# Gated attention and two mixers on one core: clamp and loads one pair further ahead, the first mixer's early weights in one piece

## The chip, the cores and the metric

One of the eight cores of one Trainium2 chip. A core has TensorE (PE in the profile; PEld is its weight load), VectorE (DVE), ScalarE (ACT), GpSimd (POOL) and SyncE (SP), which here issues all DMA transfers; they run on the core's 16 DMA engines. The metric is the time of one execution on the device in microseconds (us), median of several runs.

## The reference

A linear attention with a decay per channel, for 4 batches of 8 heads, 768 tokens, 48 channels a head, feeds two mixers:

```
f = 1 / (1 + exp(-f_logit))
for t in range(S):
    state = f[:, :, t, :, None] * state + einsum('bhd,bhe->bhde', k[:, :, t], v[:, :, t])
    y[:, :, t] = einsum('bhd,bhde->bhe', q[:, :, t], state)
x = y as [batch, token, 384]
theta = x @ w_theta
u = x + w_tok_r @ (x * cos(theta)) + w_tok_i @ (x * sin(theta))
x = u + relu(u @ w_ch)
h = relu(x @ w_in);  a, v = halves of h;  v normalised over channels
out = (a * (w_spatial @ v + b_spatial)) @ w_out
```

## The kernel before

The program has three parts, one after the other, with a barrier between them: `attention` (about the first 121 us), `token_mix` and `gated_net`. Only `attention` is changed. (A fourth, `attention_any_decay`, runs only if a flag says that the decays sum up to too much; here it is skipped.)

**Attention works on pairs of heads.** 32 heads make 16 pairs. A pair's rows (two heads of 48 channels, at partitions 0 to 47 and 64 to 111) stand over its 768 tokens, in 6 chunks of 128. A pair goes through these steps, each a function that issues instructions on one engine:

- SP: `load_f` (L231) loads the gate logits, `load_rest` k, q and v; `store` writes the pair's y from `y_sb` to the tensor `xT` in HBM.
- DVE: `keep_in_range` (L490), the clamp of `f_raw` from below. ACT: `neg_logs` (L314, L316), Exp and Ln into `csum`. DVE: `sums` (L498, L501), a copy of chunk starts and the running sum in `csum`. POOL: `sum_tops`.
- ACT: `decays` (L323, `w_dn`), `growths` (L338, `w_up`), `chunk_ends` (L330, `ends`). DVE: `scale_queries` (L516, `qs`), `scale_keys` (L527, `ks`).
- PE: `turn` (L382) transposes the keys, ACT's `keys_out` (L349) copies them out; `scores` (L400) makes the scores inside the chunks; DVE's `scores_out` (L535, `att`) masks half of them, ACT's `scores_copy` (L355) and POOL's `mask_scores` (L295) the other half; `states` (L418) makes the chunks' states, which DVE's `state_sums` (L545) scans; `attended` (L439) and `carried` (L449) add up y in PSUM; ACT's `y_out` (L362) copies it to `y_sb`.

**The order is a software pipeline written by hand.** `pipeline(eng, stages)` runs turns n = 0, 1, 2, ...; in turn n it issues for each (function, lag) of the engine's list the step of pair n - lag, in the order of the list. Turns 0 to 3 are unrolled, turns 4 to 15 are a loop over four turns each, and the rest is unrolled again. Engines issue in order and meet through semaphores: a step waits for its inputs and until its output buffer is free. `p.back(2)` in a wait is the pair that used the same of two buffers. `f_raw`, `k_raw`, `q_raw`, `csum`, `w_dn`, `w_up`, `ks`, `att` and `y_sb` have two buffers, `qs` and `v_raw` four. So `load_f` waits for the Exp two pairs back, `load_rest` for `ks` and `qs` two pairs back and y four pairs back, `y_out` for the store two pairs back.

**The first mixer's weights.** `w_raw` is a staging area for the mixers' weights, of which the first 4224 columns (theta and two sixths of the token mixing) are loaded during attention: `load_weights` (L248) issues one slice of 352 columns (176 KB) in each turn of the loop, twelve in all. With the last pair `theta_hi` on ACT waits for all of them and splits the theta weights into a high part, `theta_lo` on DVE makes the low part. The other weights are loaded by `token_mix`, 768 KB at a time.

Of the kernel before, what the change touches and what calls it, by code (L numbers as in the profile page):

```python
# [25 lines left out]
UNROLL = 4  # L26
# [13 lines left out]
WB_COLS = W_CH + DT * DMODEL  # L40

MIX_PART = 2 * SEQ
WB_EARLY = W_MIX + 2 * MIX_PART
WB_PART = WB_EARLY // (PAIRS - UNROLL)


W_IN_COLS = DT * DFF
# [63 lines left out]
def attention(nc, sems, waits_passed, flag, flag_ready, w_hi, w_lo, w_raw, wb_in, wb_hi, wb_lo, wB, qT, kT, fT, vC, xT):  # L111
# [5 lines left out]
    with ExitStack() as ctx:  # L117
# [75 lines left out]
        def last_pair(p):  # L193
            return p.reg is None and p.const == PAIRS - 1

        def pipeline(eng, stages, most=3):

            def steps(reg, consts, bounded):
                for n in consts:
                    for fn, lag in stages:  # L200
                        p = n - lag
                        if not bounded or 0 <= p < PAIRS:
                            fn(Step(reg, UNROLL, p), p % UNROLL)
            steps(None, range(UNROLL), True)
            with eng.Fori(0, PAIRS // UNROLL - 1) as it:
                steps(it, range(UNROLL, 2 * UNROLL), False)
            steps(None, range(PAIRS, PAIRS + most), True)

        def across(t, hd, c):
# [9 lines left out]
        @block.sync  # L219
        def _(sp):  # L220
            for c in x_out:
                c.open(sp)

            def rows(raw, src, name, sem, p, b):
                if p.reg is None and p.const < 2:
                    sp.wait_ge(cleared[name], b + 1)
                for hd in range(2):
                    sp.dma_start(raw[b % 2][HEAD_AT[hd]:HEAD_AT[hd] + HDIM, :],
                                 src[p.times(1), hd * HDIM:(hd + 1) * HDIM, :]).then_inc(sem[b % 2].h, 16)

            def load_f(p, b):  # L231
                sp.wait_ge(lg_done.h, lg_done.at(p.back(2), 1))
                rows(f_raw, fT, "f", f_in, p, b)

            def load_rest(p, b):
                sp.wait_ge(k_done.h, k_done.at(p.back(2), 1))
                rows(k_raw, kT, "k", k_in, p, b)
                sp.wait_ge(q_done.h, q_done.at(p.back(2), 1))
                rows(q_raw, qT, "q", q_in, p, b)
                sp.wait_ge(y_ps.h, y_ps.at(p.back(4), 2))  # L240
                sp.dma_start(v[b][:, :].rearrange("p (h x) -> p h x", h=2),
                             vC[p.times(1), :, :, :].rearrange("h p x -> p h x")).then_inc(v_in[b].h, 16)

            def load_weights(p, b):

                if p.reg is not None:
                    cols = bass.ds(p.times(WB_PART, -UNROLL * WB_PART), WB_PART)
                    sp.dma_start(w_raw[:, cols], wB[:, cols]).then_inc(wb_in, 16)  # L248

            def store(p, b):  # L250
                i = b % 2
                sp.wait_ge(y_sbd.h, y_sbd.at(p, 2))
                for hd in range(2):
                    sp.dma_start(xT[p.times(1), hd * HDIM:(hd + 1) * HDIM, :],
                                 y_sb[i][HEAD_AT[hd]:HEAD_AT[hd] + HDIM, :]).then_inc(x_out[i].h, 16)

            pipeline(sp, [(load_f, 0), (load_rest, 1), (load_weights, 0), (store, 4)], 4)
            for b in range(2):
                sp.wait_ge(x_out[b].h, 32 * (PAIRS // 2 + 1))

        @block.gpsimd
        def _(pool):
# [32 lines left out]
                    pool.affine_select(out=group, in_=group, compare_op=ALU.is_ge, fill=0.0, base=0,  # L295
                                       pattern=[[0, 3], [1, CHUNK]], channel_multiplier=-1).then_inc(a_sb.h, 1)

            pipeline(pool, [(sum_tops, 1), (mask_scores, 2)])

        @block.scalar  # L300
        def _(act):
# [37 lines left out]

            def theta_hi(p, b):  # L340
                if last_pair(p):
                    act.wait_ge(wb_in, 16 * (PAIRS - UNROLL))
                    split_hi(act, w_hi[:, W_THETA:W_MIX], w_raw[:, W_THETA:W_MIX]).then_inc(wb_hi, 1)

            def keys_out(p, b):
# [11 lines left out]
            def y_out(half):  # L357
                def f(p, b):
                    i = b % 2
                    act.wait_ge(x_out[i].h, half_count(x_out[i], p, 2) - 32)  # L360
                    act.wait_ge(y_ps.h, y_ps.at(p, half + 1))
                    act.activation(y_sb[i][:, half * 384:half * 384 + 384], y_ps_[half][0:ROWS, 0:384], ACT.Copy)\  # L362
                       .then_inc(y_sbd.h, 1)
                return f

            pipeline(act, [(neg_logs, 0), (keys_out, 2), (decays, 1), (growths, 1), (scores_copy, 2), (chunk_ends, 1), (theta_hi, 2), (y_out(0), 3), (y_out(1), 3)])

        @block.tensor
        def _(pe):
# [16 lines left out]
            def scores(half):  # L386
                def f(p, b):
                    i = b % 2
                    pe.wait_ge(q_done.h, q_done.at(p, 1))
                    pe.wait_ge(k_done.h, k_done.at(p, 1))  # L390
                    for hd in range(2):

                        if half == 0:
                            pe.wait_ge(a_masked.h, a_masked.at(p.back(1), hd + 1))
                        else:
                            pe.wait_ge(a_out.h, a_out.at(p.back(1), hd + 1))
                    for c in range(3 * half, 3 * half + 3):
                        for hd in range(2):
                            rows = slice(HEAD_AT[hd], HEAD_AT[hd] + HDIM)
                            last = pe.matmul(att_ps[2 * half + hd][:, (c % 3) * CHUNK:(c % 3 + 1) * CHUNK],  # L400
                                             ks[i][rows, c * CHUNK:(c + 1) * CHUNK],
                                             qs[b][rows, c * CHUNK:(c + 1) * CHUNK], start=True, stop=True)
                            if c % 3 == 2:
                                last.then_inc(a_ps.h, 1)
                return f
# [48 lines left out]
            def turn_tops(p, b):  # L454
                if last_pair(p):
# [3 lines left out]
                    pe.matmul(kt_ps_[0:1, 0:ROWS], top[:, :], ident[0:ROWS, 0:ROWS], start=True, stop=True)\  # L459
                      .then_inc(tops_turned, 1)  # L460

            pipeline(pe, [(turn, 2), (scores(0), 2), (scores(1), 2), (attended(0), 3), (attended(1), 3), (states, 2),
                          (carried(0), 3), (carried(1), 3), (turn_tops, 3)])
            last = Step(None, 1, PAIRS - 1)

            pe.wait_ge(a_masked.h, a_masked.at(last, 1))
# [4 lines left out]
        def _(dve):  # L471
# [57 lines left out]
            def scores_out(g):  # L529
                def f(p, b):  # L530
                    dve.wait_ge(y_ps.h, y_ps.at(p.back(2), 2))
                    dve.wait_ge(a_ps.h, a_ps.at(p, g + 1))
                    if first(p) and g == 0:
                        dve.wait_ge(const_ready, 5)
                    dve.tensor_tensor(att[b % 2][:, g * 384:(g + 1) * 384],  # L535
                                      view(att_ps[g], 0, [[CHUNK, 3], [1, CHUNK]]),
                                      view(causal, 0, [[0, 3], [1, CHUNK]]), ALU.mult).then_inc(a_masked.h, 1)
                return f
# [11 lines left out]
                    dve.wait_ge(wb_hi, 1)  # L550
                    split_lo(dve, w_lo[:, W_THETA:W_MIX], w_raw[:, W_THETA:W_MIX], w_hi[:, W_THETA:W_MIX]).then_inc(wb_lo, 1)

            pipeline(dve, [(keep_in_range, 0), (sums, 1), (scores_out(0), 2), (scores_out(1), 2), (scale_queries, 1), (scale_keys, 1), (state_sums, 2), (row_tops, 1), (theta_lo, 2)])
            dve.wait_ge(wb_lo, 1)

            dve.wait_ge(tops_turned, 1)
# [1412 lines left out]
```

## Time and profile before

| | us |
|---|---|
| median of 3 runs | 646.15 |
| lowest, highest | 645.97, 650.05 |
| the profiled execution's own time | 648.72 |
| its span, first to last instruction | 647.0 |
| PE busy over the span | 600.0 (93%) |
| DVE busy | 367.8 (57%) |
| ACT busy | 290.4 (45%) |
| mean granted clock of TensorE | 0.973 |

The profile is of one execution. Engine busy times are sums over the whole span; attention is a stage with other proportions than the mixers, and is read by itself. A row of the timeline is a run of instructions of one kind: start, duration, engine, line, output<-inputs, count, and in brackets how long the engine was idle before it and what ended that. "Us to landing" of a DMA is from its issue to the semaphore that says that it is done. The granted clock is a share of TensorE's full 2.4 GHz.

### The profile page before, as it was taken

What the parts mean: (1) busy time and instruction counts of PE and PEld (TensorE: products, weight loads), DVE (VectorE), ACT (ScalarE), POOL (GpSimd) and SP (SyncE); (2) the same over time, 40 slices, a digit from 0 to 9 for tenths busy, and PEclk for the clock granted to TensorE, in tenths of its full rate; (3) what the DMA queues carried; (4) which work ended last, traced back from release to release, by engine and by line L of the source; (5) the groups of instructions that cost most, each with busy time, mean ns of one, the idle gap of its engine ahead of it and who ended that gap; (6) DMA issues with size and microseconds to landing.
All of it is one profiled execution on the core that took longest, in us unless ns stands there. A gap on an engine that the chain in (4) does not pass through costs nothing. (4 is left out here: it accounts for less than half of the span.)

```text
span 647.0 us, 12122 instructions
## 1 busy us (share of the span) xinstructions
PE 600.0 (93%) x4262; PEld 574.4 (89%) x4262; DVE 367.8 (57%) x618; ACT 290.4 (45%) x513; POOL 31.5 (5%) x68
## 2 busy tenths in 40 slices
PE   1988989579979999999999989999999999999998
PEld 1877877469979999999999987999999899989998
DVE  6888999247677644845573363865505642463141
ACT  5877988245556323533442123632531343134112
POOL 2222223000000000000000000000000000000000
PEclk9996999969979999999999989999999999999999
DMA  8897997282041022102201413350022002000102
GB/s 187 184 255 214 252 257 198 58 291 77 25 146 50 25 62 98 37 36 64 83 12 37 146 63 135 108 162 0 2 74 74 0 0 73 0 0 14 62 0 74
DMA packets 33707, 58.77 MB, mean 91 GB/s; under 512 B 3968, under 2 KB 25984, under 8 KB 33664
## 3 DMA queue, kind: packets, MB, share of 16 engines
q1 hardware_dynamic: 33664, 58.21, 30.9%
q8 instruction: 25, 0.41, 0.3%
q14 instruction: 18, 0.15, 0.1%
HBM read 44.04 MB, written 14.16 MB: 90 GB/s over the span
## 5 line engine op out<-in xcount | busy, mean ns | idle before, releaser
L999 PE MATMUL mix_ps<-w_hi,z_hi 128*128 128x384 f32 x288 | 99.8, 346 | 2.4 <-DVE z_lo L78 2.4
L999 PE MATMUL mix_ps<-w_lo,z_hi 128*128 128x384 f32 x288 | 97.8, 340 | 0.0
L999 PE MATMUL mix_ps<-w_hi,z_lo 128*128 128x384 f32 x288 | 97.6, 339 | 0.0
L999 PE MATMUL gate_ps<-w_hi,w_lo 128*128 128x384 f32 x192 | 64.2, 334 | 0.0
L999 PE MATMUL gate_ps<-w_hi 128*128 128x384 f32 x192 | 64.1, 334 | 0.0
L999 PE MATMUL gate_ps<-w_lo,w_hi 128*128 128x384 f32 x192 | 64.1, 334 | 0.0
L999 PEld LDWEIGHTS mix_ps<-w_hi,z_hi 128*128 128x128 f32 x288 | 54.6, 190 | 3.6 <-issue 3.6
L999 PEld LDWEIGHTS mix_ps<-w_lo,z_hi 128*128 128x128 f32 x288 | 54.5, 189 | 0.0
L999 PEld LDWEIGHTS mix_ps<-w_hi,z_lo 128*128 128x128 f32 x288 | 54.4, 189 | 0.0
L73 ACT ACTIVATE g_hi<-gate 128x384 fp32r<-128x384 f32 x32 | 16.9, 527 | 76.0 <-DVE gate L1875 76.0
L1871 DVE TENSOR_TENSOR gate<-gate_ps,b_all 128x384 f32<-128x384 f32 x32 | 17.8, 557 | 56.8 <-PE gate_ps L999 56.4
L78 DVE TENSOR_TENSOR xt_lo<-xt,xt_hi 128x1152 fp32r<-128x1152 f32 x16 | 21.4, 1355 | 46.8 <-ACT xt_hi L73 46.8
L1445 DVE TENSOR_TENSOR z<-z,xn 128x384 f32<-128x384 f32 x48 | 24.7, 555 | 26.3 <-ACT z L1248 26.3
L1242 ACT ACTIVATE turns<-ang 128x384 f32<-128x384 f32 x24 | 12.7, 527 | 54.0 <-DVE ang L1433 54.0
L999 PEld LDWEIGHTS gate_ps<-w_lo,w_hi 128*128 128x128 f32 x192 | 36.0, 188 | 0.0
L999 PEld LDWEIGHTS gate_ps<-w_hi 128*128 128x128 f32 x192 | 36.0, 188 | 0.0
L999 PEld LDWEIGHTS gate_ps<-w_hi,w_lo 128*128 128x128 f32 x192 | 36.0, 188 | 0.0
L1231 ACT ACTIVATE turns<-theta_bank 128x384 f32<-128x384 f32 x24 | 11.7, 488 | 51.5 <-PE theta_bank L999 51.4
L999 PE MATMUL ringc<-xt_hi,in_hi 128*128 128x384 f32 x96 | 32.2, 336 | 0.5 <-ACT ut L1700 0.5
L999 PE MATMUL ringc<-w_hi,g_lo 128*128 128x384 f32 x96 | 32.2, 336 | 0.0
L999 PE MATMUL ringc<-w_hi,g_hi 128*128 128x384 f32 x96 | 32.2, 336 | 0.0
L999 PE MATMUL ringc<-w_lo,g_hi 128*128 128x384 f32 x96 | 32.2, 336 | 0.0
(129 smaller groups left out, 1390.1 us busy)
## 6 DMA issues: line engine op xcount, KB each, us to landing
f_raw<-in_fT_dram SPq DMA_DIRECT2D x32, 144.0 KB, 3.3
k_raw<-in_kT_dram SPq DMA_DIRECT2D x32, 144.0 KB, 3.7
q_raw<-in_qT_dram SPq DMA_DIRECT2D x32, 144.0 KB, 4.1
v_raw<-in_vC_dram SPq DMA_DIRECT2D x16, 288.0 KB, 4.5
xT<-y_sb SPq DMA_DIRECT2D x32, 144.0 KB, 2.9
xt<-xT SPq DMA_DIRECT2D x8, 576.0 KB, 4.1
u<-xT SPq DMA_DIRECT2D x8, 576.0 KB, 5.3
x2T<-x SPq DMA_DIRECT2D x24, 192.0 KB, 1.9
```

The costliest lines, as they stand in the source:

```text
L73: return act.activation(hi, x, ACT.Copy)
L78: return dve.tensor_tensor(lo, x, hi.bitcast(F32), ALU.subtract)
L999: done = pe.matmul(out, a, b, start=(first and n == 0), stop=(last and n == len(terms) - 1))
L1231: act.activation(turns[s % 2][:, :], theta_bank[:, 0:DMODEL], ACT.Copy, bias=MAGIC, scale=TURN_INV).then_inc(turns_done.h, 1)
L1242: act.activation(turns[i][:, :], ang[i][:, :], ACT.Abs).then_inc(mag_done.h, 1)
L1445: dve.tensor_tensor(z[i][:, cols], z[i][:, cols], part(xn, s * DMODEL, DMODEL), ALU.mult)\
L1871: dve.tensor_tensor(cols, gate_ps[g % 4][:, 0:HALF], part(b_all, th * HALF, HALF), ALU.add)\
```

## The change

Everything in `attention` but the loads of a pair and its clamp is issued one turn later. On DVE the clamp also leaves its place at the head of the turn and stands behind the masks of the scores. SP's loads keep their lags, its store goes from lag 4 to 5, and SP's unrolled part is eight turns long. The slices of weights leave the loop; three transfers of 1152, 1536 and 1536 columns are issued behind the loads of the last pair, ahead of a store.

```
-WB_EARLY = W_MIX + 2 * MIX_PART
-WB_PART = WB_EARLY // (PAIRS - UNROLL)
+WB_EARLY = [(W_THETA, W_MIX), (W_MIX, MIX_PART), (W_MIX + MIX_PART, MIX_PART)]
...
-        def pipeline(eng, stages, most=3):
+        def pipeline(eng, stages, most=4, lead=UNROLL):
...
-            steps(None, range(UNROLL), True)
-            with eng.Fori(0, PAIRS // UNROLL - 1) as it:
-                steps(it, range(UNROLL, 2 * UNROLL), False)
+            steps(None, range(lead), True)
+            with eng.Fori(0, (PAIRS - lead) // UNROLL) as it:
+                steps(it, range(lead, lead + UNROLL), False)
             steps(None, range(PAIRS, PAIRS + most), True)
...
             def load_weights(p, b):
-
-                if p.reg is not None:
-                    cols = bass.ds(p.times(WB_PART, -UNROLL * WB_PART), WB_PART)
-                    sp.dma_start(w_raw[:, cols], wB[:, cols]).then_inc(wb_in, 16)
+                if last_pair(p):
+                    for at, n in WB_EARLY:
+                        sp.dma_start(w_raw[:, at:at + n], wB[:, at:at + n]).then_inc(wb_in, 16)
...
-            pipeline(sp, [(load_f, 0), (load_rest, 1), (load_weights, 0), (store, 4)], 4)
+            pipeline(sp, [(load_f, 0), (load_rest, 1), (load_weights, 1), (store, 5)], 5, 2 * UNROLL)
...
-            pipeline(dve, [(keep_in_range, 0), (sums, 1), (scores_out(0), 2), (scores_out(1), 2), (scale_queries, 1), (scale_keys, 1), (state_sums, 2), (row_tops, 1), (theta_lo, 2)])
+            pipeline(dve, [(sums, 2), (scores_out(0), 3), (scores_out(1), 3), (keep_in_range, 0), (scale_queries, 2), (scale_keys, 2), (state_sums, 3), (row_tops, 2), (theta_lo, 3)])
```

The lists of ACT, PE and POOL keep their order, with each lag one higher (on ACT `neg_logs` goes from 0 to 1). `theta_hi` waits for three transfers in place of twelve.

DVE, in the unrolled turns before its loop (turn 2 before, turn 3 after); `f_raw` is the clamp, `csum` the running sum, `att` the masks of two groups of scores, `state` the scan of the states. Before:

```order
L490 TENSOR_SCALAR f_raw<-f_raw 112x768
L498 COPY cap<-csum 112x6
L501 SCALAR_TENSOR_TENSOR csum<-csum,cap 112x768
L535 TENSOR_TENSOR att<-att_ps,causal 128x384 x2
L516 TENSOR_TENSOR qs<-q_raw,w_dn 112x768
L527 TENSOR_TENSOR ks<-k_raw,w_up 112x768
L545 SCALAR_TENSOR_TENSOR state<-kv_ps,ends 112x288
L490 TENSOR_SCALAR f_raw<-f_raw 112x768
```

The same place after the change (line numbers are two lower):

```order
L496 COPY cap<-csum 112x6
L499 SCALAR_TENSOR_TENSOR csum<-csum,cap 112x768
L533 TENSOR_TENSOR att<-att_ps,causal 128x384 x2
L488 TENSOR_SCALAR f_raw<-f_raw 112x768
L514 TENSOR_TENSOR qs<-q_raw,w_dn 112x768
L525 TENSOR_TENSOR ks<-k_raw,w_up 112x768
L543 SCALAR_TENSOR_TENSOR state<-kv_ps,ends 112x288
```

Both pieces sum pair 1, mask the scores of pair 0 and scale pair 1. Before, the clamp of pair 2 stands in front of the sum and that of pair 3 behind the state scan; after, that of pair 3 stands between the masks and `qs`, and none next to the sum.

SP, from the last turn of its loop on to the end of attention; `xT` is the store, the x8 at the end are the stores of the last four pairs. Before:

```order
L241 DMA v_raw<-in_vC_dram 128x2x288
L248 ISA
L248 DMA w_raw<-in_wB_dram 128x352
L252 REGISTER_ALU
L254 DMA xT<-y_sb 48x768 x2
L205 REGISTER_ALU
L205 COMPARE_AND_BRANCH
L228 DMA k_raw<-in_kT_dram 48x768 x2
L228 DMA q_raw<-in_qT_dram 48x768 x2
L241 DMA v_raw<-in_vC_dram 128x2x288
L254 DMA xT<-y_sb 48x768 x8
```

The same place after the change:

```order
L252 DMA xT<-y_sb 48x768
L252 ISA
L252 DMA xT<-y_sb 48x768
L204 REGISTER_ALU
L204 COMPARE_AND_BRANCH
L227 DMA k_raw<-in_kT_dram 48x768 x2
L227 DMA q_raw<-in_qT_dram 48x768 x2
L240 DMA v_raw<-in_vC_dram 128x2x288
L246 DMA w_raw<-in_wB_dram 128x1152
L246 DMA w_raw<-in_wB_dram 128x1536 x2
L252 DMA xT<-y_sb 48x768 x10
```

The slices are gone, and in the unrolled end three large transfers stand between the last v and the stores of the last five pairs.

## Rows read from the trace of the kernel before

**Rows 1.** Waits of DVE, 31.4 to 105.5 us: total, times, longest

```profile
DVE qs L516 <- ACT w_dn L323: 5.2, 12, 1.1
DVE f_raw L490 <- DMA f_raw<-in_fT_dram: 2.4, 1, 2.4
DVE state L545 <- PE kv_ps L418: 1.8, 1, 1.8
DVE att L535 <- PE att_ps L400: 0.3, 1, 0.3
```

**Rows 2.** Timeline of DVE, one pair: start, duration, instruction, [idle before it]

```profile
101.15 0.69 DVE L490 TENSOR_SCALAR f_raw<-f_raw 112x768 f32<-112x768 f32 x1
101.95 1.76 DVE L501 TENSOR_TENSOR_SCAN csum<-csum,cap 112x768 f32<-112x768 f32 x1
103.63 0.99 DVE L535 TENSOR_TENSOR att<-att_ps,causal 128x384 f32<-128x384 f32 x2
104.97 0.96 DVE L516 TENSOR_TENSOR qs<-q_raw,w_dn 112x768 f32<-112x768 f32 x1 [0.35 <-ACT w_dn L323]
105.86 0.96 DVE L527 TENSOR_TENSOR ks<-k_raw,w_up 112x768 f32<-112x768 f32 x1
```

**Rows 3.** Timeline of ACT, the same pair

```profile
102.03 0.84 ACT L314 ACTIVATE csum<-f_raw 112x768 f32<-112x768 f32 x1 [0.57 <-DVE f_raw L490]
103.65 0.55 ACT L349 ACTIVATE kt<-kt_ps 128x480 f32<-128x480 f32 x1
104.11 0.83 ACT L323 ACTIVATE w_dn<-csum 112x768 f32<-112x768 f32 x1
```

**Rows 4.** Timeline of PE, the same pair: its first and its last group

```profile
100.62 0.70 PE L382 MATMUL kt_ps<-heads_first,ks 112*128 112x112 f32 x5 [0.61 <-DVE ks L527]
104.94 1.34 PE L449 MATMUL y_ps<-qs,state 48*48 48x128 f32 x20
```

**Rows 5.** Busy time by stretch; the last three columns: granted clock, DMA share, GB/s

```profile
core 0: us, PE busy (x) PEld busy (x) DVE busy (x) ACT busy (x) POOL busy (x), PEclk, DMA share, GB/s
94.25:100.50 6.25, 5.61 (x93) 4.84 (x93) 5.87 (x10) 5.64 (x11) 1.65 (x4) 1.00 1.04 264
4.00:25.50 21.50, 10.80 (x100) 9.65 (x102) 17.68 (x28) 14.88 (x23) 3.80 (x13) 1.00 1.05 223
52.00:62.00 10.00, 10.00 (x104) 8.93 (x106) 8.02 (x11) 8.30 (x15) 3.18 (x5) 0.51 0.79 213
134.00:138.00 4.00, 2.26 (x11) 1.80 (x11) 1.84 (x2) 1.44 (x2) 0.00 (x0) 0.93 0.98 376
```

**Rows 6.** DMA issues, 84 to 102 us: count, KB each, us to landing

```profile
f_raw<-in_fT_dram SPq DMA_DIRECT2D x6, 144.0 KB, 3.3
xT<-y_sb SPq DMA_DIRECT2D x6, 144.0 KB, 3.0
w_raw<-in_wB_dram SPq DMA_DIRECT2D x3, 176.0 KB, 4.3
```

**Rows 7.** Timeline: the late f_raw, TensorE behind it, a usual issue

```profile
48.86 0.56 DVE L490 TENSOR_SCALAR f_raw<-f_raw 112x768 f32<-112x768 f32 x1 [2.43 <-DMA f_raw<-in_fT_dram]
51.93 0.85 PE L418 MATMUL kv_ps<-v_raw,kt 128*48 128x48 f32 x20 [2.43 <-ACT kt L349]
96.49 0.86 SPq L228 DMA_DIRECT2D f_raw<-in_fT_dram  x2
```

**Rows 8.** Timeline: first query scaling, first masks, second turn of keys

```profile
12.12 0.96 DVE L516 TENSOR_TENSOR qs<-q_raw,w_dn 112x768 f32<-112x768 f32 x1 [1.08 <-ACT w_dn L323]
16.89 1.02 DVE L535 TENSOR_TENSOR att<-att_ps,causal 128x384 f32<-128x384 f32 x2 [0.59 <-PE att_ps L400]
19.70 1.20 PE L382 MATMUL kt_ps<-heads_first,ks 112*128 112x112 f32 x5 [0.65 <-DVE ks L527]
```

**Rows 9.** Timeline: the end of attention, copy of y for pair 13 and y's next use

```profile
112.29 0.87 ACT L362 ACTIVATE y_sb<-y_ps 112x384 f32<-112x384 f32 x2
114.52 1.52 PE L439 MATMUL y_ps<-att,v_raw 128*48 128x128 f32 x24
```

More of the change, by code:

```diff
@@ L296, in mask_scores @@
                                        pattern=[[0, 3], [1, CHUNK]], channel_multiplier=-1).then_inc(a_sb.h, 1)
-            pipeline(pool, [(sum_tops, 1), (mask_scores, 2)])
+            pipeline(pool, [(sum_tops, 2), (mask_scores, 3)])
         @block.scalar
@@ L341, in theta_hi @@
                 if last_pair(p):
-                    act.wait_ge(wb_in, 16 * (PAIRS - UNROLL))
+                    act.wait_ge(wb_in, 16 * len(WB_EARLY))
                     split_hi(act, w_hi[:, W_THETA:W_MIX], w_raw[:, W_THETA:W_MIX]).then_inc(wb_hi, 1)
@@ L364, in y_out @@
                 return f
-            pipeline(act, [(neg_logs, 0), (keys_out, 2), (decays, 1), (growths, 1), (scores_copy, 2), (chunk_ends, 1), (theta_hi, 2), (y_out(0), 3), (y_out(1), 3)])
+            pipeline(act, [(neg_logs, 1), (keys_out, 3), (decays, 2), (growths, 2), (scores_copy, 3), (chunk_ends, 2), (theta_hi, 3), (y_out(0), 4), (y_out(1), 4)])
         @block.tensor
@@ L460, in turn_tops @@
                       .then_inc(tops_turned, 1)
-            pipeline(pe, [(turn, 2), (scores(0), 2), (scores(1), 2), (attended(0), 3), (attended(1), 3), (states, 2),
-                          (carried(0), 3), (carried(1), 3), (turn_tops, 3)])
+            pipeline(pe, [(turn, 3), (scores(0), 3), (scores(1), 3), (attended(0), 4), (attended(1), 4), (states, 3),
+                          (carried(0), 4), (carried(1), 4), (turn_tops, 4)])
             last = Step(None, 1, PAIRS - 1)
```

## The prediction

> **What bounds the kernel now.** I read the page first, then windows of the first 140 us, the waits of the vector engine (DVE) there, and the timelines of one pair. Only attention (the first 121 us) is touched; what follows is the same code on the same data, so I carry it over unchanged. The profiled execution took 648.72 us, 647.0 of it the span; the median of the three runs is 646.15.
>
> In the steady loop one pair takes 6.25 us. DVE is busy nearly all of it: from the clamp at 101.15 to the key scaling at 105.86 only one gap stands, 0.35 us ahead of the query scaling, which waits for ScalarE's (ACT's) w_dn [rows 2]. So without that wait a pair costs DVE 6.25 - 0.35 = 5.90 us. Why is w_dn late? ACT is idle for 0.57 us ahead of its first Exp, waiting for the clamp of this very pair (101.15, ending 101.84); then come Exp, Ln, the copy of kt, and w_dn from 104.11 to 104.94 [rows 3]. The period is thus a loop over two engines: clamp, Exp, Ln, kt, w_dn, qs, ks, state, next clamp. ACT by itself needs 6.25 - 0.57 = 5.68 us, and TensorE, which starts its turn of keys at 100.62 and ends the carried part at 106.28, needs 5.66 and idles 0.61 [rows 4]. The order is DVE 5.90, ACT 5.68, TensorE 5.66.
>
> The DMA engines are the fourth resource. From 94.25 to 100.50 their share is 1.04 at 264 GB/s [rows 5], and a pair brings four loads, a store and a slice of weights. In the stretch shown nothing waits for them, but once in the loop a clamp did: 2.43 us for f_raw at 48.86. It opened a gap of 2.43 us on TensorE, after which [rows 7] the granted clock was 0.51 from 52 to 62, about the lower level, 1.2 GHz [rows 5]; a state scan then waited 1.8 us and a mask 0.3 us for TensorE. All waits of DVE from 31.4 to 105.5 are 5.2 + 2.4 + 1.8 + 0.3 = 9.7 us [rows 1].
>
> **The change part by part.** Numbering turns by the pair's query scaling, everything but clamp and loads keeps its order; the clamp runs a pair earlier and stands behind the score masks.
>
> 1. The ACT wait for the clamp. Exp(n) now needs a clamp of the turn before, so ACT's 0.57 us of idle goes. What is late next? w_dn needs the scan, which ends 103.71 in [rows 2]; Exp, Ln and kt (2.08 us from 102.03 to 104.11) can be done during the scan. w_dn then ends about 0.95 us after the scan, while DVE has masks (0.99) and clamp (0.69) to do before it wants it. DVE becomes the bound at 5.90. Of the 5.2 us [rows 1] the first and longest wait, 1.1 us, is at the loop's entry, where ACT was late from TensorE and not from the clamp; I keep it. Removed: 4.1 us over 11 waits. Bounds: 0, if another engine's wait takes its place at 6.25; 4.4, if the ends of instructions overlap as ks and qs do now.
>
> 2. The late f_raw and what hung on it. f_raw is now asked for behind k, q, v and a store. SyncE's next load of k waits for a key scaling; behind it go k, q, v and the store, four groups of about 0.9 us each like the one of f_raw [rows 7], so f_raw is issued some 3.5 us after that scaling ends. The clamp follows the scaling's end by a state scan and cap copy (0.6), a period (5.9) and scan and masks (2.9), 9.4 us in all: 5.9 us between issue and clamp, where now it is 96.49 to 101.15, 4.7 us [rows 7, 2]. A normal f_raw lands in 3.3 us [rows 6], so both do; a lag like the one at 48.86 would still cost, but less by 1.2 us, and with the weight slices gone (176 of 1616 KB a pair) a lag drains sooner. I take all of 2.4 + 1.8 + 0.3 = 4.5 us as gone; at the other end none of it goes.
>
> 3. The weights in the loop. At 264 GB/s a pair's 1.65 MB needs 6.25 us. Without the slice it is 1.475 MB: 5.6 us at that rate, under 5.90. The hostile row is the start, loads alone, share 1.05 at only 223 GB/s [rows 5]: 1.475 MB at that rate is 6.6 us. The nearer row is the steady one, with the same mix of loads and stores, so I take 5.6, no cost. Bounds: 0 to 0.7 us a pair.
>
> 4. The start. A third clamp stands ahead of the first qs and a fourth ahead of the second. The first qs ran at 12.12 with 1.08 us of idle before it [rows 8], so it moves by about 0.4; the mask behind it waits for TensorE, and the fourth clamp, 0.6 us, comes only after that mask. The second ks ends 0.9 us later, and TensorE's turn at 19.70 waited for exactly that [rows 8]. TensorE is the path from there until its fast stretch, so I charge 0.8 us. Bounds 0.4 and 1.4 (two clamps of 0.69).
>
> 5. The weights behind the last pair. Three DMAs, 2.16 MB, issued behind the loads of the last pair and ahead of the store of pair 11. These loads start when ks(13) is done, in today's times 100.6 (the turn of keys at 100.62 waits for it [rows 4]); three loads of 0.295 MB at 223 GB/s are through by about 104.8, the weights at the 376 GB/s of the first mixer's large weight loads [rows 5] by 110.6, or at 264 GB/s by 113.0. The store lands some 3 us after it heads the queue (3.0 in steady state [rows 6]): 113.6 to 116. ACT's copy of y for pair 13, today at 112.29, needs that y buffer free; it is followed by the last kt and mask copies. TensorE touches this y bank at 114.52 [rows 9], and the copy of the first half takes half of 0.87. So there are 1.8 us of slack, and the cost is 0 in the quick case and about 1.9 in the slow one. I take 0.2. The conversion of theta weights on ACT comes only after the mask copies and finds the weights landed.
>
> That a store is held up by loads ahead of it rests on the rows: in one burst f lands in 3.3 us, w in 4.3 [rows 6]. The Trainium skill (DMA: Bandwidth & Descriptors, "Queues, rings and completion order") says that on each DMA engine the descriptors of a queue are consumed in ring order. By that rule the store cannot overtake any part of the 2.16 MB, and term 5 is never below its quick case; if stores could overtake, it would be 0 and the forecast 0.2 us lower.
>
> 6. SyncE unrolls 8 turns rather than 4 and all engines one more at the end. Fetches of that code lie beside work as now: 0.
>
> **Sum.** 648.72 - 4.1 - 4.5 + 0.8 + 0.2 = 641.1 us. Against the median the question is whether the timed runs had the late f_raw too. If they all did, 646.15 - 7.6 = 638.5; if none did, 646.15 - 3.1 = 643.0. The spread of the timed runs, 645.97 to 650.05, lets both stand, and 641.1 lies between. It is 0.8% under the median; about 1% (6.5 us) is what a measurement of this kernel can tell from no change.
>
> **The rivals.**
> A. The late f_raw was an accident of the profiled execution, or comes again in the new kernel. Then only term 1 counts: 646.15 - 4.1 + 1.0 = 643.0. For it: f_raw waits only once in the 12 turns of [rows 1], and the issue margin grows only by 1.2 us. Against: the DMA share near 1 makes a lag last.
> B. The whole stall is systematic and gone in all runs: 638.5. For it: with a share of 1.04 there is nothing to drain a lag with. Against: at 94 to 100 us the share is the same and no load is waited for.
> C. Another wait takes w_dn's place: DMA sets the pace. At 223 GB/s a pair needs 6.6 us, over some 11 pairs 0.35 x 11 = 3.9 us more than today, plus 1.0 for start and end: 651.0, slower. It decides from the point where a pair's transfers exceed 5.9 us (250 GB/s), and turns into a loss over 6.25 (236 GB/s). Against it: 264 GB/s in the same mix.
> D. The burst of weights holds up y's copy so long that TensorE idles as it did at 51.93, 2.43 us [rows 7], and its clock falls for the last stretch. Stall 1.9 us, and the some 6.4 us of work from 114.52 to 120.9 twice as long: about +8; 646.15 - 3.1 + 8 = 651. It decides from a gap near 2.4 us; gaps of 0.61 us left the clock at 1.00 [rows 4, 5]. Against it: 1.8 us of slack.
> E. The change doesn't do what it says: ACT still arrives late, since w_dn needs the scan; nothing won, 0.8 lost: 647. Against: 0.95 us behind the scan is before DVE asks.
>
> **Chances.** Forecast 0.40, A 0.25, B 0.20, C 0.04, D 0.04, E 0.07. The forecast's own range is 639 to 642.5. For 8 in 10 I take 637.5 (B and a little) to 646.0 (short of E). The bound of faster by over 1% is 639.7: all of B and some 0.14 of the forecast, 0.34. Slower by over 1% is 652.6, reached by the worse half of C and D: 0.04. The rest, 0.62, is within 1%.
>
> **What would show it.** Right: qs starts 5.9 us apart, no DVE wait for w_dn but at the loop's entry, ACT's Exp without a wait for the clamp but with a short wait of w_dn for the scan, no f_raw wait, the clock at 1.00 from 26 to 122 us, share of DMA below 1 in the loop; the second pair's turn on TensorE at about 20.6; the store of pair 11 landing near 114 and the first stage's last copy of y some 7 to 8 us earlier than today. Wrong: periods of 6.2 with waits for f, k or q (C), TensorE at half clock or ACT idle for a y store ahead of the last copies (D), w_dn waits of 0.3 in each pair (E).

## The result, and the profile after

The changed kernel takes 641.49 us (median of 7 runs, 640.71 to 643.35) where the kernel before, run beside it, takes 646.36 (7 runs, 644.93 to 650.05): a ratio of 0.9914, 95% interval 0.9889 to 0.994. The forecast was 641.1. A second series of ten runs of the same kernel (below) gave 0.9944, interval 0.9915 to 0.9974; all 17 runs together have a median of 642.1. Medians are of the fast runs: one execution of 852 us and one of 1497 us among the variants below, and one of 680 us of the kernel before, are left out. The profiled execution took 640.71 us, 639.0 of it the span, against 648.72 and 647.0 before; 648.72 lies near the top of the range of the kernel before.

The waits of DVE in the after trace, over the same turns as [rows 1] (they now end at 97.2):

```profile
DVE f_raw L488 <- DMA f_raw<-in_fT_dram: 0.6, 1, 0.6
DVE qs L514 <- ACT w_dn L321: 0.4, 1, 0.4
```

The twelve waits for `w_dn` are one, in front of the fourth `qs`, at the start of the loop. One late `f_raw` is left here; another wait of 0.57 us, at 11.6 us, lies ahead of the first `qs`. The timeline of DVE, a little over one pair (answers to [rows 2]):

```profile
67.59 0.55 DVE L488 TENSOR_SCALAR f_raw<-f_raw 112x768 f32<-112x768 f32 x1
68.06 0.95 DVE L514 TENSOR_TENSOR qs<-q_raw,w_dn 112x768 f32<-112x768 f32 x1
68.92 0.95 DVE L525 TENSOR_TENSOR ks<-k_raw,w_up 112x768 f32<-112x768 f32 x1
69.79 0.75 DVE L543 TENSOR_TENSOR_SCAN state<-kv_ps,ends 112x288 f32<-112x288 f32 x1
...
70.79 1.76 DVE L499 TENSOR_TENSOR_SCAN csum<-csum,cap 112x768 f32<-112x768 f32 x1
72.46 1.00 DVE L533 TENSOR_TENSOR att<-att_ps,causal 128x384 f32<-128x384 f32 x2
73.38 0.55 DVE L488 TENSOR_SCALAR f_raw<-f_raw 112x768 f32<-112x768 f32 x1
73.84 0.95 DVE L514 TENSOR_TENSOR qs<-q_raw,w_dn 112x768 f32<-112x768 f32 x1
```

No idle time stands in brackets in these rows any more. From one `qs` to the next are 73.84 - 68.06 = 5.78 us (5.79 in the turns after). ACT and TensorE, two pairs after that (answer to [rows 3] and [rows 4]):

```profile
87.65 0.86 ACT L312 ACTIVATE csum<-f_raw 112x768 f32<-112x768 f32 x1
...
89.30 0.55 ACT L347 ACTIVATE kt<-kt_ps 128x480 f32<-128x480 f32 x1
89.95 0.84 ACT L321 ACTIVATE w_dn<-csum 112x768 f32<-112x768 f32 x1
```

```profile
85.57 1.34 PE L447 MATMUL y_ps<-qs,state 48*48 48x128 f32 x20
87.30 0.70 PE L380 MATMUL kt_ps<-heads_first,ks 112*128 112x112 f32 x5 [0.40 <-DVE ks L525]
```

Exp starts without the 0.57 us of waiting for the clamp. TensorE still waits for `ks`, here 0.40 us. The stretches that answer to [rows 5] (one turn, the loop, the start):

```profile
core 0: us, PE busy (x) PEld busy (x) DVE busy (x) ACT busy (x) POOL busy (x), PEclk, DMA share, GB/s
85.42:91.21 5.79, 5.39 (x101) 4.86 (x98) 5.76 (x9) 5.66 (x11) 2.00 (x3) 1.00 0.97 254
28.00:95.00 67.00, 62.25 (x1070) 56.14 (x1070) 65.53 (x91) 64.29 (x114) 21.89 (x33) 1.00 0.90 242
4.00:25.50 21.50, 9.94 (x88) 8.80 (x90) 17.54 (x28) 15.22 (x23) 3.92 (x13) 1.00 0.96 223
```

The granted clock is 1.00 through the loop, and DVE is busy 65.53 of 67 us. Start and end of attention (answers to [rows 8] and [rows 9], DVE, TensorE and ACT apart):

```profile
12.11 0.96 DVE L514 TENSOR_TENSOR qs<-q_raw,w_dn 112x768 f32<-112x768 f32 x1
19.15 1.27 DVE L525 TENSOR_TENSOR ks<-k_raw,w_up 112x768 f32<-112x768 f32 x1
```

```profile
20.56 1.19 PE L380 MATMUL kt_ps<-heads_first,ks 112*128 112x112 f32 x5 [1.52 <-DVE ks L525]
```

```profile
105.44 0.87 ACT L360 ACTIVATE y_sb<-y_ps 112x384 f32<-112x384 f32 x2 [1.38 <-DMA xT<-y_sb]
```

The first `qs` did not move (12.12 before). The second turn of keys on TensorE is 0.86 us later than before (20.56 against 19.70), 0.32 us of it for the long `ks`, and ACT's copy of y for pair 13 now waits 1.38 us for the store of pair 11.

**Where the 8 us of the profiled executions come from.** Marks on DVE's `qs`: the fourth is at 31.33 before and 32.47 after (+1.14, the start); from the fourth to the fifteenth, eleven turns, 73.64 us before and 64.20 after. Taking out the stall of 4.5 us before, and the late `f_raw` (0.57) with the long `ks` behind it (0.32) after, eleven ordinary turns take 69.1 and 63.3: -5.8. The stall gives -4.5 + 0.9 = -3.6. From the last `ks` to the first mixer's loads of x it takes 18.28 us before (111.34 to 129.62) and 18.58 after (103.01 to 121.59): +0.3. Sum 1.14 - 5.8 - 3.6 + 0.3 = -8.0. The rest of the program takes 517.4 us in both.

Three remarks on these terms. Of the -5.8, eleven periods shorter by 0.46 us are 5.1; 0.33 is the fifteenth turn, which has no clamp any more since the clamps run a pair ahead (5.46 us from the fourteenth `qs` to the fifteenth); the rest is turns of the kernel before that took more than 6.25 us. The 1.14 belongs to these two executions: the fourth `qs` is at 31.84 in the second profile of the kernel before and at 31.81 in that of the changed kernel (both kernels are run once more below), so the start varies by 0.5 to 0.7 us in one kernel. And the +0.3 at the end can't be told from nothing, since the second profile of the kernel before takes 18.60 us there.

### The profile page after: what moved, and what is told of

Read it like the earlier page. It is cut to its first block and busy times, and to the rows that moved or that the text cites. A ratio compares the mean times of both kernels' runs of the same rounds, so it can differ in the third digit from the quotient of the medians.

```text
span 639.0 us, 12023 instructions
## 1 busy us (share of the span) xinstructions
PE 594.3 (93%) x4262; PEld 571.2 (89%) x4262; DVE 367.5 (58%) x618; ACT 290.2 (45%) x513; POOL 35.8 (6%) x68
```

## The experiments

**The slices of weights stay in the loop.** The changed kernel, but the twelve slices of 176 KB are loaded in turns 4 to 15 again. It parts the shift of the pipeline from the move of the weights.

```diff
-                if last_pair(p):
-                    for at, n in WB_EARLY:
-                        sp.dma_start(w_raw[:, at:at + n], wB[:, at:at + n]).then_inc(wb_in, 16)
+                if p.reg is not None or UNROLL <= p.const < 2 * UNROLL:
+                    at = p.times(WB_PART, -UNROLL * WB_PART)
...
+                    sp.dma_start(w_raw[:, cols], wB[:, cols]).then_inc(wb_in, 16)
```

> The changed kernel with the twelve weight slices of 176 KB back in the turns 4 to 15, nothing else. Theory (the pair's pace is set by DVE at 5.8 us now, and the DMA engines move about 264 GB/s in the old kernel's mix): a pair then brings 1.65 MB, which needs 6.25 us at that rate, so the loop falls back to about 6.2 us a pair with waits of the clamp for f_raw of some 0.4 us each; 641.5 + 11 x 0.4 = 646, no better than the old kernel. Rival (DMA has room, 264 GB/s was only what was asked for): no DMA waits, periods of 5.8 us, 641.5 to 642.5.

Measured: 642.79 us (10 runs), ratio 0.9934, 0.9911 to 0.9957. The ordinary turns took 5.79 us until 63 us and 6.12 from 69 to 94. In that stretch:

```profile
69.00:94.00 25.00, 21.98 (x385) 19.79 (x381) 24.59 (x34) 23.15 (x43) 7.96 (x12) 1.00 1.06 270
```

A share of 1.06 and a period of 6.12 look like the DMA engines setting the pace. But nobody waits for a transfer in this stretch. What is longer is one instruction of DVE, `ks`, in all five turns, and what POOL does beside it:

```profile
81.31 0.95 DVE L515 TENSOR_TENSOR qs<-q_raw,w_dn 112x768 f32<-112x768 f32 x1
82.18 1.27 DVE L526 TENSOR_TENSOR ks<-k_raw,w_up 112x768 f32<-112x768 f32 x1
```

```profile
82.00 1.82 POOL L294 TENSOR_SCALAR_AFFINE_SELECT att<-att 128x384 f32<-128x384 f32 x2 [1.72 <-ACT att L354]
```

POOL's select starts 0.18 us ahead of `ks`, and `ks` takes 1.27 us in place of 0.95. An `f_raw` was late once in the loop, 0.74 us at 50.9. The shift alone, with the slices in the loop, brings as much of the gain as the intervals can tell: rival C does not hold at these rates. My 646 missed.

**The burst alone.** The kernel before, but the weights are loaded in three transfers behind the last pair's loads; no stage is moved.

```diff
-            pipeline(sp, [(load_f, 0), (load_rest, 1), (load_weights, 1), (store, 5)], 5, 2 * UNROLL)
+            pipeline(sp, [(load_f, 0), (load_rest, 1), (load_weights, 1), (store, 4)], 4)
```

(and all other lists as before the change)

> The old kernel with only the weights moved behind the last pair's loads. Theory (two separate gains: the wait of w_dn for the clamp, 4.1 us, and the late f_raw with what hangs on it, up to 4.5 us, which comes from the DMA share of 1.04): DVE keeps waiting 0.35 us a pair for w_dn and periods stay 6.25 us, but the late f_raw goes: profile about 644, and timed runs 1 to 4 us under the old kernel's. Rival A (the late f_raw is an accident): timed runs equal the old kernel's within 1 us. DMA share in the loop falls to about 0.95.

Measured: 646.76 us (10 runs), ratio 1.0, 0.9974 to 1.0025. DVE's waits:

```profile
DVE qs L514 <- ACT w_dn L321: 6.4, 13, 1.1
```

The wait for `w_dn` is as it was, the period 6.25, and no `f_raw` is late in this profile. The emptier loop is worth nothing that the timed runs can tell (the interval is 1.6 us to either side), as under rival A; my 1 to 4 us missed.

**The clamp at the head of DVE's turn.** The changed kernel with the clamp ahead of the sum.

```diff
-            pipeline(dve, [(sums, 2), (scores_out(0), 3), (scores_out(1), 3), (keep_in_range, 0), (scale_queries, 2), ...
+            pipeline(dve, [(keep_in_range, 0), (sums, 2), (scores_out(0), 3), (scores_out(1), 3), (scale_queries, 2), ...
```

> The changed kernel with the clamp back at the head of DVE's turn, still one pair ahead of the Exp. Theory (what counts is that the Exp needs a clamp of an earlier turn; the place in the turn only sets how long f_raw may take): no w_dn waits, period 5.8 us, but f_raw has 2.9 us less to land, 3 us instead of 5.9, which is under the 3.3 us that it takes: waits of the clamp for f_raw in most turns, 0.3 to 1.5 us each, 645 to 652. Rival (loads settle themselves earlier as SyncE waits only for an Exp that is now early): within 1 us of the changed kernel.

Measured: 654.76 us (4 runs), ratio 1.0104, 1.0048 to 1.0161, the slowest of all variants.

```profile
DVE f_raw L488 <- DMA f_raw<-in_fT_dram: 11.9, 6, 4.5
DVE state L543 <- PE kv_ps L416: 5.3, 4, 1.5
```

The clamp is asked for some 2.6 us earlier in its turn (in the rows of the changed kernel, from the scan at 70.79 to the clamp at 73.38), and that is slack which `f_raw` had: it is late six times, TensorE idles, and the granted clock over 28 to 95 us is 0.90. The longest of these waits, 4.5 us, lies ahead of the first `qs`, which comes at 15.76 rather than 12.11; that is 3.6 us of the 13. The place in the turn, as much as the lag of a pair, makes the change work.

**The kernel before, once more.**

> The old kernel again, one look. If the late f_raw and the clock at the lower level behind it are systematic (rival B), this profile shows a wait of DVE for f_raw of 1 to 3 us once between 30 and 70 us; if an accident (rival A), none, and the attention stage ends some 4 us earlier than 121.

Measured: 647.19 us in one execution. The profile:

```profile
DVE qs L516 <- ACT w_dn L323: 6.4, 13, 1.1
...
DVE f_raw L490 <- DMA f_raw<-in_fT_dram: 1.4, 2, 1.2
```

A late `f_raw` comes again, in the same turn as in [rows 7] and half the size (1.21 us at 48.22, and 0.22 at 40.80), and without a fall of the clock in attention (1.00 over 28 to 95 us). Over the three turns around it that costs 1.6 us where it cost 4.5, and attention ends 2.3 us earlier than in the first profile. This is between my two cases: the stall of [rows 7] was an accident in its size, while that the same turn is late again speaks against an accident altogether. Two profiles, and the one of the burst alone without a late `f_raw`, do not say how usual it is.

**Slices of twice the size.** As the first experiment with slices of 352 KB, 1.835 MB a pair. It loads twice as many weights early, which the mixer loads once more; what is computed stays.

```diff
+WB_PART = 704
```

> As the run with the slices kept in the loop, but with twelve slices of 352 KB (further weights into staging space that is loaded again later). It looks for the point from which the DMA engines set the pace. With slices of 176 KB (1.65 MB a pair) the loop held its pace of 5.8 us. A pair now brings 1.835 MB. Theory (the engines are near their end at some 285 GB/s): 6.4 us a pair, waits for f_raw, k or q of 0.5 us or more in most turns, 646 to 650. Rival (share 1.06 is no limit yet): periods of 5.8 us, 642 to 644.

This text says that with 176 KB the loop "held its pace"; it did only until 63 us, as told above. Measured: 646.25 us (10 runs), ratio 0.9998, 0.997 to 1.0027. `f_raw` is late four times (2.5 us in all, 0.6 of it ahead of the first `qs`), the period lies between 5.8 and 8.1:

```profile
31.40:105.50 74.10, 67.84 (x1096) 61.29 (x1096) 68.66 (x93) 66.13 (x119) 22.00 (x35) 0.93 0.94 276
```

Here transfers do cost: the granted clock fell too, to a mean of 0.93 in this stretch.

**A longer burst.** The changed kernel with two more transfers of 768 KB behind the last pair's loads (the mixer loads these weights once more; what is computed stays).

```diff
-WB_EARLY = [(W_THETA, W_MIX), (W_MIX, MIX_PART), (W_MIX + MIX_PART, MIX_PART)]
+WB_EARLY = [(W_THETA, W_MIX), (W_MIX, MIX_PART), (W_MIX + MIX_PART, MIX_PART),
+            (W_MIX + 2 * MIX_PART, MIX_PART), (W_MIX + 3 * MIX_PART, MIX_PART)]
```

> The changed kernel with a burst of five transfers (3.74 MB) in place of three (2.16 MB) behind the last pair's loads; the two more fill staging space that the first mixer loads again. Theory (the store of pair 11 waits its turn behind the burst, ACT's copy of y for pair 13 behind the store, and 1.8 us of slack cover that, of which 1.4 us are used now): 1.57 MB at 376 GB/s are 4.2 us more, so ACT waits 5.6 us for the store and the end of attention moves by 3.8 us; if TensorE's clock falls behind that gap some 5 us more: 645 to 651. Rival (stores overtake loads, or the slack is larger): under 642.5.

Measured: 648.45 us (10 runs), ratio 1.0035, 1.0008 to 1.0062. ACT, TensorE, and the stretch with its granted clock:

```profile
111.08 0.87 ACT L361 ACTIVATE y_sb<-y_ps 112x384 f32<-112x384 f32 x2 [8.11 <-DMA xT<-y_sb]
```

```profile
111.71 2.80 PE L438 MATMUL y_ps<-att,v_raw 128*48 128x128 f32 x24 [6.54 <-ACT y_sb L361]
```

```profile
108.00:116.00 8.00, 4.29 (x58) 4.25 (x60) 0.67 (x1) 3.14 (x6) 0.99 (x2) 0.57 0.23 75
```

The chain of term 5 and rival D, link by link: the store of pair 11 is held up behind the burst, ACT waits for the y buffer, TensorE idles 6.54 us, and its granted clock is then 0.57, about the lower level (1.2 GHz), so the group takes 2.80 us where it took 1.52. From the last `ks` (101.92) to the loads of x (128.7) are 26.8 us, 8.2 more than in the changed kernel, for 6.7 us more of waiting. The store is two transfers, one for each head. The burst's last transfer, issued at 97.01, lands after 13.3 us, at 110.3; the store's first, issued behind it at 97.90, lands after 10.0 us, at 107.9, and only the second after it, at 111.1, when ACT starts. I had expected ACT to wait 5.6 us and not 8.11. Against the 3.66 us of the changed kernel's second profile (below) the two more transfers add 4.45 us, near the 4.2 us that I had worked out for them; what I had taken for the wait without them, 1.4 us, was a quick case.

**The store of pair 11 ahead of the burst.**

```diff
-            pipeline(sp, [(load_f, 0), (load_rest, 1), (load_weights, 1), (store, 5)], 5, 2 * UNROLL)
+            pipeline(sp, [(load_f, 0), (load_rest, 1), (store, 5), (load_weights, 1)], 5, 2 * UNROLL)
```

> The changed kernel with the store of pair 11 issued ahead of the burst. Theory (the wait of 1.4 us of ACT's y copy for that store lies inside the slack): the wait is gone from the profile and the time stays the same, 641 to 642. Rival (the wait cost something): 1 us faster.

Measured: 640.9 us (10 runs), ratio 0.9901, 0.9872 to 0.9929. The copy of y waits no more:

```profile
103.01 0.87 ACT L360 ACTIVATE y_sb<-y_ps 112x384 f32<-112x384 f32 x2
```

From the last `ks` to the loads of x are 18.3 us, as in the kernel before. The median lies 0.1 us under the 641 to 642 of my theory and 0.6 us under the 641.49 of the changed kernel, where the rival had 1 us: the runs do not part them.

**The changed kernel, once more.**

> The changed kernel once more, for a second profile. If its time in the loop is set by DVE's own work, the period between two qs is again 5.79 us in the turns without a late f_raw, and the time is 641.5. If the scaled keys (ks) take 1.27 us whenever POOL's select happens to start more than 0.1 us before them, some turns of this profile show 1.27 and others 0.95, since in the first profile the two starts lay within 0.02 us of each other. Waits of DVE for f_raw: 0 to 2.5 us in all, in other turns than the first time.

Measured: 642.63 us (10 runs, 638.28 to 645.31). Every ordinary turn is 5.79 us again, `f_raw` is late once, 0.9 us at 11.95, ahead of the first `qs`, and never in the loop; apart from the second and third turn `ks` keeps 0.95. The news is at the end of attention: ACT, TensorE, the stretch with its granted clock, and the transfer's time to landing:

```profile
106.27 0.87 ACT L360 ACTIVATE y_sb<-y_ps 112x384 f32<-112x384 f32 x2 [3.66 <-DMA xT<-y_sb]
```

```profile
106.91 2.24 PE L437 MATMUL y_ps<-att,v_raw 128*48 128x128 f32 x24 [2.10 <-ACT y_sb L360]
```

```profile
104.00:114.00 10.00, 7.87 (x118) 7.13 (x116) 3.03 (x4) 4.13 (x8) 1.00 (x2) 0.83 0.28 85
```

```profile
w_raw<-in_wB_dram SPq DMA_DIRECT2D x1, 768.0 KB, 9.8
```

The burst's last transfer lands 9.8 us after its issue, rather than 8.4 in the first profile, and the same small wait is now 3.66 us. TensorE idles 2.10 us and its granted clock is 0.83 over the next ten. From the last `ks` (101.57) to the loads of x (123.56) are 22.0 us: this execution gives back 3.7 us of what the loop won.

**The clamp on POOL**, between its copy of the tops and its select; DVE loses it.

```diff
-            pipeline(pool, [(sum_tops, 2), (mask_scores, 3)])
+            pipeline(pool, [(sum_tops, 2), (keep_in_range, 0), (mask_scores, 3)])
```

> The changed kernel with the clamp on POOL between its two tasks, where it has some 3.5 us idle a pair. Theory (DVE is the bound at 5.8 us with ACT at 5.7 and TensorE at 5.66 just behind): DVE falls to 5.3 us, ACT becomes the bound at 5.7, so only 0.1 us a pair and 0.4 at the start are won: 640 to 641, if POOL's clamp takes under 2 us. Rival (POOL's clamp takes longer or slows DVE's instructions beside it, as POOL's selects and DVE's key scaling already lengthen each other): 643 or more.

Measured: 641.83 us (11 runs), ratio 0.9928, 0.99 to 0.9956. The profiled execution (636.88) is the lowest of the eleven, with a period of about 5.65 us and the fourth `ks` at 30.45 rather than 33.36: TensorE's early groups were quick one turn sooner (the scores at 20.85 us took 1.61 us, those at 21.68 of the changed kernel 2.93). In two later profiles with this clamp the fourth `ks` is at 33.23 and 33.44, so that part belongs to this execution and not to the clamp. POOL's clamp takes 2.13 us, more than the 2 us that my theory allowed, and `qs` beside it 1.07 to 1.26 us rather than 0.95. No gain over the changed kernel can be told.

**The clamp behind `ks`.** The changed kernel, clamp moved from ahead of `qs` to behind `ks`.

```diff
-... (keep_in_range, 0), (scale_queries, 2), (scale_keys, 2), (state_sums, 3), ...
+... (scale_queries, 2), (scale_keys, 2), (keep_in_range, 0), (state_sums, 3), ...
```

> The clamp moved from the place ahead of the cap to the place behind ks. ks then starts about 0.47 us earlier against POOL's select. Theory of the two engines' shared reading (ks is slow when POOL's select has begun before it): every ks takes 0.95 us, the clamp itself may now lie beside the select and take 0.61 to 0.69 us, the period is 5.8 to 5.9 us and steady, and the time 641 to 643. Rival (the length of ks has to do with DMA traffic, as the slices that stay in the loop lengthened it too): ks keeps both lengths, 0.95 and 1.27, and the time is that of the changed kernel or 2 us above it. f_raw is needed 1.0 us or more later in the turn, so its waits should vanish under both.

Measured: 643.47 us (9 runs), ratio 0.9968, 0.9948 to 0.9989. DVE and POOL in a turn:

```profile
69.78 0.96 DVE L525 TENSOR_TENSOR ks<-k_raw,w_up 112x768 f32<-112x768 f32 x1
70.65 0.88 DVE L488 TENSOR_SCALAR f_raw<-f_raw 112x768 f32<-112x768 f32 x1
71.45 0.74 DVE L543 TENSOR_TENSOR_SCAN state<-kv_ps,ends 112x288 f32<-112x288 f32 x1
```

```profile
70.13 1.78 POOL L293 TENSOR_SCALAR_AFFINE_SELECT att<-att 128x384 f32<-128x384 f32 x2 [1.72 <-ACT att L353]
```

The select now starts 0.35 us behind `ks`, and `ks` is short in every turn of the loop. The one long `ks` (1.27 us) is in the third turn, where the select began 0.07 us ahead of it. The clamp lies beside the select and costs 0.80 us from start to start where it cost 0.47. That is more than the 0.61 to 0.69 I expected, the period is 6.07 to 6.24, and the time is above my range though `f_raw` is never late. That the order of the two starts decides the length of `ks` came out as foreseen; the price for the clamp was too low.

**The clamp on POOL and the store first.**

> The clamp on POOL and the store of pair 11 ahead of the burst, together. Each alone gave 640.9 and 641.8. If each part's gain is real and they add, the loop runs at 5.65 us a pair (1.5 us less over 11 pairs), the wait of 2.2 us for y_sb goes, and the time is 638 to 639.5. If POOL is then the engine that is late (its turn is 2.1 us longer), nothing is gained and the time is 640 to 642.

Measured: 641.27 us (8 runs), ratio 0.9928, 0.9901 to 0.9954. The wait for y is gone, but the timed runs show no sum of the two gains. In the profiles attention does end earlier, with the loads of x at 119.65 against 120.41 for the store first alone; the rest of the program took 519.9 us in this execution and 515.9 in that one, more than what is looked for. In one turn `f_raw` was 0.3 us late for POOL, so POOL's clamp slid beside the scalings of DVE:

```profile
54.56 2.13 POOL L302 TENSOR_SCALAR f_raw<-f_raw 112x768 f32<-112x768 f32 x1 [0.32 <-DMA f_raw<-in_fT_dram]
```

```profile
54.71 1.49 DVE L519 TENSOR_TENSOR qs<-q_raw,w_dn 112x768 f32<-112x768 f32 x1
56.12 1.26 DVE L530 TENSOR_TENSOR ks<-k_raw,w_up 112x768 f32<-112x768 f32 x1
```

**The clamp on POOL and the slices in the loop**, so that the loop is quick and the transfers are many.

> The clamp on POOL, and the weights' slices of 176 KB back in the loop: 1.65 MB a pair at a DVE period of 5.65 us asks for 292 GB/s. If 264 to 268 GB/s is the limit of this mix of transfers, the period is 6.1 to 6.2 us, DVE and POOL wait for f_raw and PE or ACT for keys and values (more than 4 us in all), and the time is 643 to 645. If there is no such limit and what lengthened the loop with the slices was the slow ks alone, every ks takes 0.95 us, the period is 5.65 to 5.8 us with next to no waits for transfers, and the time is 638 to 641.

Measured: 642.93 us (9 runs), ratio 0.994, 0.9913 to 0.9968. Between 62.5 and 96.2, about six turns, and POOL's waits from 28 to 124:

```profile
62.50:96.20 33.70, 31.61 (x542) 28.46 (x539) 33.30 (x42) 32.93 (x60) 20.39 (x24) 1.00 1.03 284
```

```profile
POOL f_raw L303 <- DMA f_raw<-in_fT_dram: 1.6, 3, 1.2
```

The same transfers as in the kernel before, at 284 GB/s over 33.7 us with turns of 5.5 to 6.2 us. Of the three late `f_raw` one, of 0.25 us, lies in this stretch, the long one of 1.2 us is at 50.2. No other load is waited for. So 264 GB/s was not what these engines can do, it was what a period of 6.25 us asks for. The median, though, is above the 638 to 641 that I expected without a limit, and only just under the 643 to 645 of a limit: the profile settles the rate, the timed runs don't show a gain from it.

## Why the prediction was right

The number was 0.4 us off the first series and 1.0 off the median of all 17 runs, with the mechanisms of terms 1 and 5 confirmed. The order of the causes was not: I had term 2 (-4.5) ahead of term 1 (-4.1), and measured were -3.6 and -5.8. The terms by themselves:

**Term 1, the wait for `w_dn`** (-4.1): right in mechanism. The wait went in every turn but one at the start of the loop, DVE became the bound, and the shift alone (slices left in) brings the gain, the burst alone none. It was mis-sized: the period is 5.79, not 5.90, and the turns gave -5.8 us, 0.33 of it because the fifteenth turn lost its clamp, which I had not counted. I had kept the clamp at 0.69 us; it takes 0.55 in its new place. At its old place it lay beside the end of POOL's select (0.69 us at 101.15 in [rows 2]; the select of that turn runs from 99.96 for 1.46 us, to 101.42). From the trace of the kernel before, POOL:

```profile
99.96 1.46 POOL L295 TENSOR_SCALAR_AFFINE_SELECT att<-att 128x384 f32<-128x384 f32 x2 [2.07 <-ACT att L355]
```

The clamp of [rows 7], held up by its load until the select was over, took 0.56 us. Between masks and `qs`, its new place, POOL is idle. From start to start that is 0.61 before and 0.47 after, which is the difference of the periods, 5.90 and 5.79, but for 0.03 us.

**Term 2, the late `f_raw`** (-4.5): -3.6 in the profiles, but the second profile of the kernel before shows 1.4 us of waiting and no fall of the clock, and the burst alone, without a late `f_raw` in its profile, was no faster. Between rivals A and B, nearer A. After the change the loop has one late `f_raw` of 0.57 us in one profile and none in the other. The margin grew by less than I had worked out: from issue to clamp the rows show 5.2 to 5.7 us (68.17 to 73.38, 85.07 to 90.75), not 5.9, and `f_raw` lands in 3.7 us in the median of 34 to 90 us, not 3.3. How much of this term the timed runs hold is not shown. Their medians fell by 4.9 and 3.2 us; terms 1, 4 and 5 by themselves, as measured, give -4.4 us in the first profile of the changed kernel and -1.5 in the second (start +0.5, turns -5.7, end +3.7, against the first profile before).

**Term 3, the weights out of the loop** (0): right in its result, wrong in its premise. I read a share of 1.04 at 264 GB/s as the limit. The same mix moved 284 GB/s with a share of 1.03 when the loop asked for it. Rival C rested on the same reading and on the start's 223 GB/s, and fell. Transfers cost with slices of twice the size (276 GB/s, with waits); where between these two the limit lies, and what besides the rate sets it, stays open.

**Term 4, the start** (+0.8): 1.14 in the first profile. The turn of keys came at 20.56, near what was foreseen, but by another sum: the first `qs` did not move by 0.4, it kept its place (12.11), since its wait of 1.08 us had room for the clamp; and 0.32 of the 0.86 is a long `ks` (1.27 us at 19.15, the select of POOL running since 0.33 us before it), which was no part of the working. The added 0.3 came later, from TensorE. A group of it took longer than in the kernel before:

```profile
23.69 2.09 PE L439 MATMUL y_ps<-att,v_raw 128*48 128x128 f32 x24
24.54 2.80 PE L437 MATMUL y_ps<-att,v_raw 128*48 128x128 f32 x24
```

In the second profiles the same group took 2.59 us before and 1.87 after, so this part is of the execution, not of the change; the granted clock reads 1.00 over 20 to 28 us in all four, and what makes the group longer stays open.

**Term 5, the burst and the store of pair 11** (+0.2, bounds 0 and 1.9): the mechanism stands link by link, but for one word of the prediction: that the store cannot overtake any part of the burst. One half of it landed ahead of the burst's last transfer (107.9 against 110.3 us with the longer burst); what holds is that ACT needs both halves, and the second came last. The slack was 1.6 us, not 1.8 (in two traces the wait of ACT less the idle time of TensorE: 3.66 - 2.10 and 8.11 - 6.54). A wait of 1.38 us, inside that slack, cost nothing that can be told from the spread (18.58 against 18.28 and 18.60). The one of 3.66 is just my slow case, in which ACT waits 1.8 + 1.9 us; but it cost 3.7 and not 1.9, since after a gap of 2.10 us TensorE's granted clock fell. So rival D, which I had let decide from a gap near 2.4 us at a chance of 0.04, happened in small in one of two profiles of the changed kernel. It was the lowest-priced term and the one that varied most, 3.4 us between two profiles of one kernel.

**The sum** came out since errors of both signs met: in the first profile term 1 gave 1.7 us more than forecast, term 2 gave 0.9 less, start and end cost 0.4 more. Against the timed medians it is luckier still: 646.15 less the 4.4 us of terms 1, 4 and 5 as measured in the first profile is 641.8, without any of term 2. That the forecast lay within 1 us of the medians is thus partly luck; what was right in it is why the wait for `w_dn` goes and what comes next.

**A better version?** The store first has the lowest median (640.9 against 642.1 for all runs of the change), and its trace shows the wait removed for the price of one swapped entry. The intervals of the two ratios overlap, so it is not shown to be faster, only to be free of a known risk.

## What to carry to other kernels

Shift a stage back by a pair only with a look at what its consumer's place in the turn leaves for the load: one list entry (clamp first or clamp behind the masks) was worth 13 us here, 3.6 of them at the start. A DMA share near 1 says that transfers are in flight, not that the engines are at their limit; ask whether anyone waits, and raise the demand to see. And a large transfer in the queue ahead of a small store belongs behind it, unless the time to the buffer's next use exceeds the burst's worst landing, not its median one: with the store behind the same burst the wait was between 0.2 and 3.7 us in five profiles.

## What the runs showed of the hardware

I had not expected that VectorE instructions change their length with what POOL does. With the clamp on DVE, `ks`, an instruction with two inputs from SBUF, takes 0.95 us alone, or when POOL's select starts up to 0.02 us ahead of it or later. It takes 1.27 us when the select has started 0.07 us or more before it (the changed kernel, the slices that stay, the double slices, and the clamp behind `ks` alike). The clamp costs 0.47 us from start to start by itself and 0.80 beside the select. In most turns of the changed kernel both start together, within 0.02 us (in the others the select starts 0.06 to 0.13 us later), and the select takes 1.81 us where it takes 1.46 when it starts 0.35 us behind `ks`:

```profile
68.91 1.81 POOL L293 TENSOR_SCALAR_AFFINE_SELECT att<-att 128x384 f32<-128x384 f32 x2 [1.72 <-ACT att L353]
```

so any small delay of DVE costs 0.32 us more in that turn, as it did at 57.18 behind the late `f_raw`. Transfers are not the cause: with the clamp on POOL and the slices in the loop, at 284 GB/s, `ks` took 0.95 us in five of six turns. With POOL's clamp beside DVE the order of select and `ks` is not the whole of it: three `ks` took 1.26, 1.26 and 1.61 us (the one at 56.12 above among them) though the select started behind them, each behind a late clamp on POOL, while others that POOL's clamp overlapped about as long took 0.95. What decides there stays open. The Trainium skill (GPSIMD Engine Reference, "8. Key points") states that POOL shares its SBUF interfaces with VectorE, with contention for instructions that run in a 2-port mode or have two SBUF inputs. The trace agrees for `ks`, which has two SBUF inputs (0.95 to 1.27 us). The clamp has one input and was lengthened too (0.47 to 0.80 us); that fits the sentence if the clamp runs in a 2-port mode, which no row here shows. That the order of the two starts decides for `ks` is what the runs add. Which rule of arbitration lies behind that was not tried.
